# Attention with clustered keys, then two feed-forward layers: cluster scores turned by plain transposes, their two parts summed by VectorE

## The reference

```
q, k, v: (2, 8, 768, 64)   centroids: (8, 16, 64)
q_assign = argmax_c( q_n . c_n )        k_assign = argmax_c( k_n . c_n )
scores = where(q_assign == k_assign, q k^T / 8, -1e9)
attn = softmax(scores);  x = attn v     -> (1536, 512)
x = mixture of 8 experts (one per token, relu), scaled by two gates
g = piecewise(x @ w_in);  out = g @ w_out
```

## Time and profile before

| | |
|---|---|
| median of 3 runs | 839.55 us (839.29 to 839.87) |
| the profiled execution | 839.41 us |
| its span | 837.6 us |
| TensorE busy | 801.6 us (96%) |
| VectorE busy | 450.6 us (54%) |
| ScalarE busy | 383.2 us (46%) |
| GpSimd busy | 348.0 us (42%) |

### The profile page before, as it was taken

The page is one execution under the profiler, slowest core; times in us unless marked ns, Lnnn a source line. Parts: engine busy times, 40 slices in busy tenths (PEclk is TensorE's granted clock), DMA queues, the critical chain, the costliest instruction groups (busy, mean ns, idle before and its releaser), DMA issues.

```text
span 837.6 us, 13745 instructions
## 1 busy us (share of the span) xinstructions
PE 801.6 (96%) x4370; PEld 677.3 (81%) x4371; DVE 450.6 (54%) x795; ACT 383.2 (46%) x757; POOL 348.0 (42%) x343
## 2 busy tenths in 40 slices
PE   7999999999999949999999999989999999999994
PEld 4898999999999727888888888868888888888883
DVE  5788888888888865221221221234455444554442
ACT  4788888888788744222322322212222322332222
POOL 7345654455632028778767767764000100010001
PEclk9999999999999969999999999999999999999998
DMA  4344333423121148699669669682000100010001
GB/s 108 108 123 162 98 116 88 125 57 122 47 61 23 57 154 278 223 336 382 204 241 359 215 241 348 230 287 83 1 1 1 50 1 1 0 51 1 1 0 51
DMA packets 45429, 105.44 MB, mean 126 GB/s; under 512 B 5200, under 2 KB 12880, under 8 KB 44368
## 3 DMA queue, kind: packets, MB, share of 16 engines
q1 hardware_dynamic: 29584, 60.92, 22.5%
q0 software_dynamic: 15808, 44.04, 15.6%
HBM read 92.37 MB, written 6.29 MB: 118 GB/s over the span
## 4 chain that ended last, share of the span: by engine, by line
PE 89%; DVE 3%; ACT 2%; DMA 2%; issue 1%; POOL 1%; DVEq 0%; ACTq 0%; POOLq 0%
PE ps L1493 15%; PE ps L1480 15%; PE ps L1440 13%; PE ps L1420 11%; PE ps L1245 7%; PE ps L1261 4%; PE ps L1231 4%; PE ps L1232 4%; PE ps L1259 4%; PE ps L1273 2%; PE ps L1185 2%; PE ps L1430 2%; DMA raw_w<-in_moe_w 2%; PE ps L1205 2%; PE ps L1196 1%
## 5 line engine op out<-in xcount | busy, mean ns | idle before, releaser
L394 POOL TENSOR_TENSOR weights<-raw_w,weights 128x2048 fp32r<-128x2048 f32 x34 | 157.1, 4622 | 49.2 <-DMA weights<-in_moe_w 35.3
L1493 PE MATMUL ps<-weights,g_t 128*128 128x512 f32 x576 | 141.2, 394 | 2.5 <-DVE g_t L1151 2.5
L1480 PE MATMUL ps<-y_t,weights 128*128 128x512 f32 x576 | 139.3, 391 | 0.0
L1493 PEld LDWEIGHTS ps<-weights,g_t 128*128 128x128 f32 x576 | 107.3, 188 | 27.3 <-DVE g_t L1151 4.1
L1480 PEld LDWEIGHTS ps<-y_t,weights 128*128 128x128 f32 x576 | 108.1, 188 | 23.8
L923 DVE TENSOR_TENSOR p_t<-ps,p_t 128x384 fp32r<-128x384 f32 x192 | 98.9, 550 | 27.4 <-ACT p_t L629 27.0
L1420 PE MATMUL ps<-weights,x_t 128*128 x456 | 111.1, 399 | 1.7 <-DVE x_t L1084 1.7
L1440 PE MATMUL ps<-weights,h_t 128*128 x456 | 109.6, 396 | 2.3 <-issue 1.7
L565 POOL DMA_INDIRECT out<-y_sb,order_u x12 | 11.8, 979 | 240.3 <-ACT y_sb L776 238.4
L760 ACT ACTIVATE ps<-g_a,half 128x512 f32<-128x512 f32 x48 | 33.2, 692 | 149.7 <-DVE g_b L1146 149.7
L1420 PEld LDWEIGHTS ps<-weights,x_t 128*128 128x128 f32 x456 | 85.2, 190 | 20.0 <-issue 2.4
(11 more groups left out here) (178 smaller groups left out, 1076.4 us busy)
## 6 DMA issues: line engine op xcount, KB each, us to landing
raw_w<-in_moe_w SPq DMA_DIRECT2D x32, 1024.0 KB, 6.2
weights<-in_moe_w POOLq DMA_DIRECT2D x28, 1024.0 KB, 9.1
qk_t<-qk_t SPq DMA_DIRECT2D x32, 192.0 KB, 2.6
raw_w<-in_moe_w_in SPq DMA_DIRECT2D x4, 1024.0 KB, 6.0
weights<-in_moe_w_in POOLq DMA_DIRECT2D x4, 1024.0 KB, 7.8
raw_w<-in_moe_w_out SPq DMA_DIRECT2D x4, 1024.0 KB, 7.9
weights<-in_moe_w_out POOLq DMA_DIRECT2D x4, 1024.0 KB, 12.7
raw<-in_q SPq DMA_DIRECT2D x16, 192.0 KB, 2.9
```

The costliest lines, as they stand in the source:

```text
L394: pool.tensor_tensor(weights[:, unit % 2, 1, c * CHUNK:(c + 1) * CHUNK], low_chunk(unit, c), high_chunk(unit, c).bitcast(F32), ALU.subtrac ...
L1480: last = mm(ps[:, 4 + n % 2, :], wi[:, a, k, f * P:(f + 1) * P], y_ts[g % 2][:, b, k, :], start=(k == 0 and j == 0), stop=(k == KC - 1 and ...
L1493: last = mm(ps[:, t, :], g_t[:, n % 2, a, t * P:(t + 1) * P], wo[:, b, f, :], start=(f == 0 and j == 0), stop=(f == FC2 - 1 and j == 2))
```

## The change

`cluster_rows` turns each tile by a transpose with the identity, and both parts arrive in PSUM: 128 columns a tile, in which each of the tile's four groups (query or key tiles) has two parts of 16 clusters. VectorE has a new step, `sum_scores`, that reads PSUM and writes the sums to `cs` in SBUF. The highest score and the comparison read `cs`. `fold` and its instruction go. `CL_PH` is 5. GpSimd's candidates still wait for the comparison (now count 3), and TensorE's next write to bank 7 waits for the sum (count 1) in place of the comparison (count 2). ScalarE's and SyncE's lists stay as they are, apart from line numbers.

```diff
-CL_PH = 4
+CL_PH = 5
-    fold = place("fold", [P, 4, NC], F32, small)
+    cs = place("cs", [P, 2 * QT, NC], F32, small)
-        cs_ps = ps[:, 7, 0:GW].rearrange("p (t n) -> p t n", n=P)[:, :, 0:4 * NC]\
-            .rearrange("p t (a c) -> p t a c", c=NC)
+        cs_ps = ps[:, 7, 0:GW].rearrange("p (a s c) -> p a s c", s=2, c=NC)
...
-                pool.wait_ge(cl_done, CL_PH * h + 2)
+                pool.wait_ge(cl_done, CL_PH * h + 3)
...
-            dve.tensor_tensor(fold[:], by_copy[:, :, 0], by_copy[:, :, 1], ALU.add).then_inc(const_dve, 1)
...
+            def sum_scores(h):
+                dve.wait_ge(cs_done, h + 1)
+                dve.tensor_reduce(cs[:], cs_ps.rearrange("p a s c -> p a c s"), AX.X, ALU.add).then_inc(cl_done, 1)
             def highest_score(h):
-                dve.wait_ge(cs_done, h + 1)
-                dve.tensor_reduce(cmax[:].rearrange("p (t a) -> p t a", a=4), cs_ps, AX.X, ALU.max)\
-                    .then_inc(cl_done, 1)
+                dve.wait_ge(cl_done, CL_PH * h + 1)
+                dve.tensor_reduce(cmax[:], cs[:], AX.X, ALU.max).then_inc(cl_done, 1)
             def best_clusters(h):
-                dve.wait_ge(cl_done, CL_PH * h + 1)
-                dve.tensor_tensor(by_tile(ceq[:]), cs_ps,
-                                  by_tile(cmax[:].unsqueeze(2).broadcast_to([P, 2 * QT, NC])),
+                dve.wait_ge(cl_done, CL_PH * h + 2)
+                dve.tensor_tensor(ceq[:], cs[:], cmax[:].unsqueeze(2).broadcast_to([P, 2 * QT, NC]),
                                   ALU.is_ge).then_inc(cl_done, 1)
...
-                        if s == 5 and ahead >= 2:
-                            (highest_score, best_clusters)[t](h + 2)
+                        if s == 5 and ahead >= 2 and t == 0:
+                            sum_scores(h + 2)
+                            highest_score(h + 2)
+                        elif s == 5 and ahead >= 2:
+                            best_clusters(h + 2)
...
                 for t in range(HALF):
-                    last = mm(x_ps[:, t * P:t * P + 4 * NC], ct_sb[:, t * P:(t + 1) * P],
-                              fold[:].rearrange("p i c -> p (i c)"), start=True, stop=True)
+                    last = tr(x_ps[:, t * P:(t + 1) * P], ct_sb[:, t * P:(t + 1) * P], ident[:])
                 last.then_inc(cs_done, 1)
...
-                        operands(h + 2, 0, (cl_done, CL_PH * (h + 1) + 2))
+                        operands(h + 2, 0, (cl_done, CL_PH * (h + 1) + 1))
```

More of the change, by code:

```diff
@@ L822, in _ @@
             dve.wait_ge(const_pool, 11)
-            by_copy = ident[:].rearrange("p (i s c) -> p i s c", s=2, c=NC)
-            dve.tensor_tensor(fold[:], by_copy[:, :, 0], by_copy[:, :, 1], ALU.add).then_inc(const_dve, 1)
             dve.tensor_tensor(back_w[:, :, 0:D], ident[:, 0:D].unsqueeze(1).broadcast_to([P, 2, D]),
                               ident[:, D:].unsqueeze(1).broadcast_to([P, 2, D]), ALU.add).then_inc(const_dve, 1)
-            def by_tile(ap):
-                return ap.rearrange("p (t a) c -> p t a c", a=4)
+            def sum_scores(h):
+                dve.wait_ge(cs_done, h + 1)
+                dve.tensor_reduce(cs[:], cs_ps.rearrange("p a s c -> p a c s"), AX.X, ALU.add).then_inc(cl_done, 1)
             def highest_score(h):
-                dve.wait_ge(cs_done, h + 1)
-                dve.tensor_reduce(cmax[:].rearrange("p (t a) -> p t a", a=4), cs_ps, AX.X, ALU.max)\
-                    .then_inc(cl_done, 1)
+                dve.wait_ge(cl_done, CL_PH * h + 1)
+                dve.tensor_reduce(cmax[:], cs[:], AX.X, ALU.max).then_inc(cl_done, 1)
             def best_clusters(h):
-                dve.wait_ge(cl_done, CL_PH * h + 1)
-                dve.tensor_tensor(by_tile(ceq[:]), cs_ps,
-                                  by_tile(cmax[:].unsqueeze(2).broadcast_to([P, 2 * QT, NC])),
+                dve.wait_ge(cl_done, CL_PH * h + 2)
+                dve.tensor_tensor(ceq[:], cs[:], cmax[:].unsqueeze(2).broadcast_to([P, 2 * QT, NC]),
                                   ALU.is_ge).then_inc(cl_done, 1)
@@ L846, in one_hot @@
             def one_hot(h):
-                dve.wait_ge(cl_done, CL_PH * h + 3)
+                dve.wait_ge(cl_done, CL_PH * h + 4)
                 dve.tensor_tensor(onehot[:].rearrange("p t (a r) -> p t a r", a=4)[:, :, :, 0:NC],
@@ L853, in clusters @@
             def clusters(h):
-                for step in (highest_score, best_clusters, highest_label, one_hot):
+                for step in (sum_scores, highest_score, best_clusters, highest_label, one_hot):
                     step(h)
@@ L949, in _ @@
                 rowmax(0, c)
+            sum_scores(1)
             highest_score(1)
@@ L1201, in cluster_rows @@
                 pe.wait_ge(ct_copied, h + 1)
-                if isinstance(h, int) and h == 0:
-                    pe.wait_ge(const_dve, 2)
                 for t in range(HALF):
-                    last = mm(x_ps[:, t * P:t * P + 4 * NC], ct_sb[:, t * P:(t + 1) * P],
-                              fold[:].rearrange("p i c -> p (i c)"), start=True, stop=True)
+                    last = tr(x_ps[:, t * P:(t + 1) * P], ct_sb[:, t * P:(t + 1) * P], ident[:])
                 last.then_inc(cs_done, 1)
@@ L1270, in outputs_back @@
                 if first:
-                    pe.wait_ge(const_dve, 3)
+                    pe.wait_ge(const_dve, 2)
                 for c in range(HALF):
```

## The result

The changed kernel takes 841.47 us (median of 20 runs, 840.36 to 842.96), the kernel before 839.66 us (median of 20, 838.55 to 841.99). The ratio is 1.0022, 95% interval 1.0015 to 1.0028: slower by 0.15 to 0.28%, about 1.8 us. The forecast was 841.6. The profiled execution took 841.53 us, its span 839.8, against 839.41 and 837.6.

A forecast was written before the change was run, and what follows sets the result against it. TensorE, 89% of the chain, was taken as the bound, with VectorE coming last once per head at the normalisation. Terms 1.3, 0, 0.48 and 0.4 gave +2.2 us on 839.41: 841.6 us, range 837.3 to 846.5.

The forecast's parts named there:

- TensorE saves 0.44 us a head: From cluster rows to the second score matmul after them, TensorE would take 0.51 us instead of 0.95.
- The sum takes 0.555 us: VectorE's added reduce of 384 PSUM elements, priced by length from two reduces, would take 0.555 us per head.
- the upper bound of 0.84: Rival: the sum's strided PSUM reads are slow, 0.84 us, adding 4.5 us for 846.1 us; chance 0.21.
- SBUF reads save 15 ns and the highest score starts 0.10 earlier: On VectorE after the sum: maximum 342 ns against 357, and 0.10 us of waiting gone through the earlier semaphore.
- a = 0.48: VectorE's added time per head: 0.595 - 0.015 - 0.10 = 0.48 us; a rival had it nearer 0.37, 839.9 us, chance 0.23.
- The second correction halves TensorE's lead: Step 5's second correction frees a PSUM bank late, cutting TensorE's lead at the next transposes from 0.44 to about 0.2 us.
- VectorE takes the lead at the normalisation: VectorE would reach the second normalisation 0.24 us later at a loop turn, delaying TensorE's value matmul as much; unbroken unchanged.
- The slack comes in two kinds, by the loop's jump: VectorE's wait before the second normalisation: 0.47 to 0.49 us at eight unbroken head changes, mean 0.22 at five loop turns.
- The bare chains ahead of the loop: Two cluster chains before the loop, each -0.39 for transposes and +0.595 - 0.015 for the sum: 2 x 0.19 = 0.4 us.
- my five turns at 0.26 and seven at nothing: Head changes at five loop turns would cost 0.48 - 0.22 each, 1.3 us together; unbroken ones 0.
- The 0.48 into head 14: The change into head 14 has 0 slack on VectorE, so the whole added 0.48 us would be lost there.
- my sum of 2.2: All terms together, over loop turns, unbroken changes, head 14 and the start: +2.2 us for the kernel.

The follow-up runs named there:

- the two kernels on the stride: Sum of neighbouring PSUM columns in the changed kernel: reduce 548 against 549 ns; extra reduce from SBUF at 64-byte stride in the kernel before: 565 against 557 ns.
- the turns of four heads: Changed kernel with VectorE's loop of six turns of two heads written as three turns of four heads: 840.63 us, ratio 1.001.
- the loop written out: Kernel before with VectorE's loop written out, nothing else changed: 838.91 us, ratio 0.9994.
- normalisation first: Changed kernel with VectorE's second normalisation placed ahead of the copy of the queries' one-hot in step 1: 839.77 us, ratio 0.9999.
- both edits: Changed kernel with the second normalisation ahead of the one-hot copy in step 1 and VectorE's loop written out: 837.92 us, ratio 0.9981.

## Why the prediction was right

Point by point:

- **TensorE saves 0.44 us a head:** 0.39 measured at the shown head. Without the sum 0.42 us of it reached the time of an unbroken head.
- **The sum takes 0.555 us:** 549 ns. The estimate by length from two contiguous reduces held; the upper bound of 0.84, which carried a fifth of the chance, took L1000's extra 71 ns for the price of a stride, and the two kernels on the stride show that it is not.
- **SBUF reads save 15 ns and the highest score starts 0.10 earlier:** 353 ns against 357, so only 4 ns, and 0.47 against 0.56 us. Up to the one-hot the added time was 0.49 us where a = 0.48 had been worked out; up to the normalisation it was 0.52. By the fixed costs on the Trainium skill's page "VectorE: DVE Perf Modes", section The TRN2 errata, a would have been an estimated 0.37 us. The trace does not bear that out: the highest score took 353 ns from SBUF and 357 from PSUM, the comparison 350 and 348.
- **The second correction halves TensorE's lead:** 0.39 less 0.23 leaves 0.16 us (0.2 expected).
- **VectorE takes the lead at the normalisation:** no wait left at any head change, a gap of 0.47 us ahead of the value matmul where there were 0.27. From the first correction of step 5 to the second normalisation VectorE takes 6.32 us at a turn (6.37 at head 4) and 6.07 where unbroken, against 6.01 to 6.04 before at all of them (into head 14 it is 6.07 against 5.68). That is +0.28 to 0.35 at a turn, where the sum had 0.26, and +0.04 to 0.06 where unbroken, where it had nothing: the place and the order of the terms are right, both sizes somewhat low.
- **The slack comes in two kinds, by the loop's jump:** shown twice, by the turns of four heads and by the loop written out.
- **The bare chains ahead of the loop:** TensorE got the first one-hot at 15.55 instead of 14.89 us, but 0.42 of that stood there before the first transposes (L1196 at 10.48 for 10.06; in the traces of the other experiments it starts anywhere from 10.06 to 10.47); the rest is 0.24, and 0.25 for the second (27.57 for 26.66, less the 0.66 carried over), against 0.19 each.

The parts in the profile, as the attention stage's 1.70 us: 0.24 + 0.25 in the two bare chains, 0.05 up to head 1, 1.07 for the twelve changes up to head 13, 0.48 into head 14, and -0.39 behind it. Two of these need a word.

The 1.07 look like my five turns at 0.26 and seven at nothing, and that is luck. The stretches from correction to normalisation, where the change acts, add up to 1.92 (1.55 at the turns, 0.37 at the others). The rest of the heads, from normalisation to next correction, gives 0.85 back, mostly by single longer stretches: the kernel before has 11.83 and 11.61 us among its usual 11.24 to 11.36, the changed kernel has one of 11.58, and one of only 11.01 at its first head.

The 0.48 into head 14 came as forecast, but 0.39 of them return within head 14, and the forecast had not counted that. Before, VectorE waited 0.51 us for ScalarE's copy ahead of the corrections of the next step (273.85, 2.71 us after the normalisation); now they stand 2.32 us after it (275.97) with no wait. So this term is worth 0.09, not 0.48.

The stage's 1.70 and the 0.42 ahead of it make most of the 2.2 us by which the spans of the two profiled executions differ. So that this equals my sum of 2.2 is partly luck: two terms too low and one too high by 0.39, single long heads, and a start that came late by chance. The medians differ by 1.8.

What was incomplete is the list of places. I named two where TensorE waits for VectorE; there are three. The third, step 1's transposes behind step 0's corrections, should cost nothing extra in the changed kernel, because the normalisation comes later still; I argue that from the order and did not test it. In the run with normalisation first it cost 2 us.

## What to carry to other kernels

Work taken from the busiest engine and put on one with a low mean share is paid at the few places where that engine comes last, so measure the idle time between the moved work and the next thing the busy engine waits for, and subtract. Here about 0.5 us of new work met 0.48 us of slack at most heads and 0.22 at the others, and a saving of 0.4 us a head became a loss. When a wait is moved away, look at once for the next one in the same chain: with normalisation first the turn of a loop, which had been free in the kernel before, was the bound, and only with both edits did the kernel with the transposes come out below the kernel before (how much of that the edits would give without the transposes was not run).

## What the runs showed of the hardware

A turn of VectorE's hardware loop cost about 0.25 us between its last instruction and the next (0.53 us from one-hot to correction at a turn, 0.27 to 0.28 where unbroken), filed in the rows as a wait of 0.17 us for ScalarE or as "issue". A reduce of pairs of fp32 took 548 ns from adjacent PSUM columns, 549 ns from columns 64 bytes apart, and 565 ns at that distance from SBUF. For 3 us near the start of one execution TensorE's granted clock was 0.50, and the chain of head 1's clusters came 1.4 us later than worked out; the traces of the eleven other kernels have 1.00 at that place.
